# First loads of 128 partitions in the order of need, from two queues, and the first pair's splits in pieces with part of them on GpSimd

## The chip, the cores and the metric

The kernel runs on one core of a Trainium2 chip. The metric is the device time of one execution in microseconds (us), lower is better; a time stands for the median of several runs.

## What is computed

Attention over 4 batches of 8 heads with 576 positions and head size 64, then two feed-forward layers over the 2304 tokens:

```python
scores = scale * q @ k.T                      # 576 x 576 for each head
thresh = max(scores, axis=-1) - tau
scores = where(scores >= thresh, scores, -1e9)
attn = exp(scores - max(scores)); attn = attn / (sum(attn) + 1e-09)
x = attn @ v                                  # heads side by side: 2304 x 512
for w_in, w_out, act in layer 1, layer 2:     # 512 x 2048, 2048 x 512
    h = x @ w_in
    g = h - tanh(h)   (layer 1)   or   h * sigmoid(h)   (layer 2)
    x = g @ w_out
```

All data is float32. To keep precision at the rate of the `fp32r` form, every matmul operand is split into two parts: "hi", a copy that ScalarE rounds to `fp32r`, and "lo", the raw value minus hi.

## The kernel before, in words

**Attention.** The 32 heads are worked in 16 pairs (4 pairs a batch). A pair has 9 tiles of queries (`TILES`): tiles 0 to 7 hold 128 queries of one head each, heads in turn (tile 0 is head 0, tile 1 head 1, tile 2 head 0 again), tile 8 the last 64 queries of both heads. `steps(B, ks, first)` exists on TensorE, VectorE, ScalarE and GpSimd; it walks step numbers `k`, and what belongs to tile `q` happens at a fixed lag behind (`L_S` = 8 for the scores, `L_EXP` = 9, `L_SUM` = 10, `L_NORM` = 11, `L_T` = 13 for the transposes). These lags are the hand-written order of the work.

For each tile, TensorE computes the scores (L718: k_lo then k_hi, each over two halves of 288 keys, four matmuls; tile 8 has eight) into one of two PSUM buffers. VectorE reads them twice: a pass that scales and takes the row's maximum (L552), the statistics (L568) and the pass that applies the threshold (L584, which increments `lift_done` and so frees the scores' buffer). ScalarE takes the exponential (L421), VectorE the sum's reciprocal (L561, L577), GpSimd multiplies (L346), TensorE transposes the tile (L740), ScalarE copies that to SBUF (L407), and TensorE multiplies by v (L683).

**Where keys and queries come from.** They lie in HBM with the 64 features of a head first. Each raw tile `k_raw[u]`, `q_raw[u]` has 128 partitions: the same 64 rows twice, since the stationary operand `q_parts[u]` holds q_hi in partitions 0 to 63 and q_lo in 64 to 127, against k_hi or k_lo in both halves. The source holds the 64 rows once, so SyncE (SP in the profile) loads every raw tile by two DMAs of 64 partitions: `load_first` (L280) for the first pair, head by head, keys before queries, and `load_qk` (L273) for the later pairs, both heads in one. The load of tau (L264) goes ahead of them all. `load_qk` of pair 2 waits until the first pair is split (`qk_split`).

**The split of keys and queries.** In the steps of a pair its successor's keys and queries are split: hi on ScalarE (L432, L434), k_lo (L352) and q_lo (L361, partitions 64 to 127 alone) on GpSimd. The first pair has nobody before it: ahead of its steps ScalarE makes k_hi and q_hi of head 0, then of head 1 (L438, L439), each head after all four DMAs of that head, and VectorE makes k_lo and q_lo in the same order (L591, L595). Each of these eight instructions covers all 576 positions. Ahead of them VectorE computes a handful of constants from tau (L521 to L531). TensorE waits for the two lo parts of a head (`qk_split` at 2, then at 4) before tile 0 and tile 1:

```python
            for h in range(2):
                dve.wait_ge(k_hi_done, h + 1)
                dve.tensor_tensor(k_lo[0][:, h], ...).then_inc(qk_split, 1)
                dve.wait_ge(q_hi_done, h + 1)
                dve.tensor_tensor(rows, ...).then_inc(qk_split, 1)
```

**The layers.** Weights come in by 32 DMAs (L305) and are split on ScalarE, VectorE and GpSimd. Tokens go through in chunks of 512 (the last of 256); for each chunk and layer TensorE makes 16 hidden tiles (L761) and projects them (L777), three matmuls for each product of two split operands. ScalarE applies the activation (L471, L474), VectorE forms and splits g (L614, L619, L621). The output leaves at the end of each chunk of layer 2.

## Time and profile before

| | before |
|---|---|
| median of 3 runs | 1100.23 us (1100.09 to 1100.81) |
| the profiled execution's own time | 1100.23 us |
| its span (first to last instruction) | 1098.4 us |
| PE, PEld busy | 1076.1 us (98%), 870.5 us (79%) |
| DVE, ACT, POOL busy | 559.1 us (51%), 402.8 us (37%), 265.5 us (24%) |
| DMA | 46.38 MB, mean 42 GB/s |

PE is TensorE's matmuls, PEld its weight loads, DVE VectorE, ACT ScalarE, POOL GpSimd, SP SyncE. The profile's times are microseconds from the start of the span; 1.83 us of the execution lie outside the span. The 16 attention pairs take about the first 305 us, the two layers the rest.

### The profile page before, as it was taken

To read this page: it belongs to the slowest core of one execution; us is meant where nothing else is said; L and a number is where in the kernel's file an instruction comes from. 1 tells how busy PE (TensorE), PEld (TensorE's weight loads), DVE (VectorE), ACT (ScalarE), POOL (GpSimd) and SP (SyncE) were. 2 spreads that over 40 slices of the span, in tenths; PEclk is the share of its full clock that TensorE was granted. 3 is DMA by queue.
4 is the path that set the end of the run, shared out by engine and by line. 5 is a ranking of instruction groups with operands and counts; after the bars stand their busy time and mean duration, and the time that the engine had idled before them with its cause. 6 is when DMAs were issued, how large, how long until landed. Compare 5 with 4: busy or idle time off the path is not lost.

```text
span 1098.4 us, 15693 instructions
## 1 busy us (share of the span) xinstructions
PE 1076.1 (98%) x5808; PEld 870.5 (79%) x5808; DVE 559.1 (51%) x1342; ACT 402.8 (37%) x830; POOL 265.5 (24%) x240
## 2 busy tenths in 40 slices
PE   5999999999999999999999999999999999999998
PEld 4667677676678888888888889888888888888898
DVE  7999999999767543343343344622322322222222
ACT  5889898888732211121121121422211211111111
POOL 3767676776254200000000000444000000000000
PEclk9999999999999999999999999999999999999999
DMA  6334242431142100000000000232100000010010
GB/s 153 81 74 111 57 111 66 102 89 36 58 147 96 58 1 1 1 0 0 0 0 0 0 1 1 89 111 70 39 1 1 28 10 0 0 38 0 0 39 20
DMA packets 15195, 46.38 MB, mean 42 GB/s; under 512 B 2080, under 2 KB 2592, under 8 KB 15136
## 3 DMA queue, kind: packets, MB, share of 16 engines
q1 hardware_dynamic: 15136, 45.62, 14.8%
q8 instruction: 34, 0.56, 0.2%
q14 instruction: 25, 0.20, 0.1%
HBM read 40.89 MB, written 4.72 MB: 42 GB/s over the span
## 4 chain that ended last, share of the span: by engine, by line
PE 95%; DVE 1%; ACT 1%; POOL 0%; issue 0%; DVEq 0%; ACTq 0%
PE hid L761 36%; PE acc L777 35%; PE scores L718 9%; PE pv L683 8%; PE tps L740 6%; DVE x_lo L605 0%; ACT w_parts L450 0%; ACT x_hi L459 0%; DVE probs L584 0%; DVE probs L552 0%; ACT pT L407 0%; POOL q_parts L361 0%; DVE w_parts L635 0%; DVE stats L568 0%; ACT pR L409 0%
## 5 line engine op out<-in xcount | busy, mean ns | idle before, releaser
L761 PE MATMUL hid<-x_hi,w_parts 128*128 128x512 f32 (+1 forms) x1280 | 384.9, 368 | 3.2 <-DVE x_lo L605 2.1
L777 PE MATMUL acc<-g_hi,w_parts 128*128 128x512 f32 (+1 forms) x1280 | 384.1, 368 | 0.0
L761 PEld LDWEIGHTS hid<-x_hi,w_parts 128*128 128x128 f32 x1280 | 234.2, 189 | 44.6 <-DVE x_lo L605 2.2
L777 PEld LDWEIGHTS acc<-g_hi,w_parts 128*128 128x128 f32 x1280 | 234.1, 189 | 39.9
L761 PE MATMUL hid<-x_lo,w_parts 128*128 128x512 f32 (+1 forms) x640 | 235.4, 368 | 0.0
L777 PE MATMUL acc<-g_lo,w_parts 128*128 128x512 f32 (+1 forms) x640 | 235.4, 368 | 0.0
L619 DVE CAST g_hi<-h_act 128x512 fp32r<-128x512 f32 (+1 forms) x160 | 71.2, 445 | 270.0 <-ACT h_act L474 267.3
L374 POOL TENSOR_TENSOR w_parts<-w_raw,w_parts 128x1024 fp32r<-128x1024 f32 x30 | 73.6, 2457 | 400.0 <-ACT w_parts L450 399.9
L614 DVE TENSOR_TENSOR h_act<-hid,h_act 128x512 f32<-128x512 f32 (+1 forms) x80 | 51.0, 638 | 200.8 <-ACT h_act L471 200.8
L471 ACT ACTIVATE h_act<-hid 128x512 f32<-128x512 f32 (+1 forms) x80 | 44.4, 555 | 293.3 <-PE hid L761 293.3
L474 ACT ACTIVATE h_act<-hid 128x512 f32<-128x512 f32 (+1 forms) x80 | 44.4, 555 | 290.0 <-PE hid L761 290.0
L777 PEld LDWEIGHTS acc<-g_lo,w_parts 128*128 128x128 f32 x640 | 120.7, 189 | 19.9
L761 PEld LDWEIGHTS hid<-x_lo,w_parts 128*128 128x128 f32 x640 | 120.6, 189 | 19.9
L346 POOL TENSOR_SCALAR probs<-probs,rinv 128x576 f32<-128x576 f32 x144 | 107.4, 750 | 87.5 <-DVE rinv L577 78.4
L621 DVE TENSOR_TENSOR g_lo<-h_act,g_hi 128x512 fp32r<-128x512 f32 (+1 forms) x160 | 125.1, 782 | 5.5
L552 DVE TENSOR_SCALAR_CACHE_REDUCE probs<-scores,fine 128x576 f32<-128x576 f32 x144 | 116.8, 811 | 11.6 <-PE scores L718 11.3
L718 PE MATMUL scores<-k_lo,q_parts 128*128 128x288 f32 x336 | 106.8, 341 | 14.4 <-DVE q_parts L595 9.6
L718 PEld LDWEIGHTS scores<-k_lo,q_parts 128*128 128x128 f32 x336 | 64.0, 193 | 68.3 <-issue 39.7
L584 DVE SCALAR_TENSOR_TENSOR probs<-scores,stats,probs 128x576 f32<-128x576 f32 x144 | 117.8, 818 | 0.1
L421 ACT ACTIVATE probs<-probs,stats 128x576 f32<-128x576 f32 x144 | 111.2, 772 | 5.7 <-DVE probs L584 5.3
L407 ACT ACTIVATE pT<-tps 128x512 f32<-128x512 f32 x144 | 85.7, 595 | 31.5 <-PE tps L740 30.6
L740 PE MATMUL tps<-ident,probs 128*128 128x128 f32 x656 | 97.0, 276 | 0.0
(46 smaller groups left out, 765.9 us busy)
## 6 DMA issues: line engine op xcount, KB each, us to landing
w_raw<-w_in SPq DMA_DIRECT2D x32, 512.0 KB, 3.4
k_raw<-k_in SPq DMA_DIRECT2D x30, 288.0 KB, 4.8
q_raw<-q_in SPq DMA_DIRECT2D x30, 288.0 KB, 5.9
v_all<-v_in SPq DMA_DIRECT2D x16, 320.0 KB, 3.1
out<-xT SPq DMA_DIRECT2D x4, 1024.0 KB, 4.2
k_raw<-k_in SPq DMA_DIRECT2D x4, 144.0 KB, 3.0
q_raw<-q_in SPq DMA_DIRECT2D x4, 144.0 KB, 2.9
out<-xT SPq DMA_DIRECT2D x1, 512.0 KB, 2.9
```

Source lines behind the costliest of these rows:

```text
L346: pool.tensor_scalar(tile, tile, r, 1.0, ALU.mult, ALU.mult).then_inc(norm_done, 1)
L374: pool.tensor_tensor(w_parts[f][:, 1], w_raw[f % 2][:], w_parts[f][:, 0].bitcast(F32), ALU.subtract).then_inc(w_split, 1)
L407: last = act.activation(dst, src, ACT.Copy)
L421: act.activation(tile, tile, ACT.Exp, bias=stats[:, c, 0:1], scale=-SCALE / FINE, accum_out=rowsum[:, c:c + 1]).then_inc(exp_done, 1)
L552: dve.tensor_scalar(tile, scores[q % SBUFS][:, :, 0:HALF], fine[:], None, ALU.mult, ALU.max, accum_out=finemax[:, c:c + 1]).then_inc(max_d ...
L584: dve.scalar_tensor_tensor(out=tile, in0=scores[q % SBUFS][:, :, 0:HALF], scalar=stats[:, c, 1:2], in1=tile, op0=ALU.is_lt, op1=ALU.subtra ...
L621: dve.tensor_tensor(g_lo[s][:, 0:w], g, g_hi[s][:, 0:w].bitcast(F32), ALU.subtract).then_inc(g_split, 1)
L683: last = pe.matmul(pv[h * DH:(h + 1) * DH, 0:HALF], v_of(u, c, h), keys[c][h], start=(c == 0), stop=(c == FULL))
L718: last = pe.matmul(scores[q % SBUFS][:, a, c0:c0 + w], rows, keys, start=(i == 0), stop=(i == len(todo) - 1))
L740: last = pe.matmul(bank[:, c, :], block, ident[:], is_transpose=True, start=True, stop=True)
L761: last = pe.matmul(hid[f % HBANKS][:, 0:w], a, b[:, kc, 0:w], start=(kc == 0 and i == 0), stop=(kc == KC - 1 and i == 2))
L777: last = pe.matmul(acc[n][:, 0:w], a, b[f % GRING][:, 0:w], start=(f == 0 and i == 0), stop=(f == FT - 1 and i == 2))
```

## The change

What it does:

- The source arrays of keys and queries hold the 64 feature rows twice (`np.concatenate([rows, rows])` on the host), and every load of keys or queries is one DMA of 128 partitions instead of two of 64. This holds for all 16 pairs.
- The first pair's keys are loaded head by head by SyncE, and its queries in four pieces: the first 128 positions of head 0, the first 192 of head 1 (its layout has the last 64 queries in front), then the rest of head 0 (448) and of head 1 (384). The first piece and tau are loaded from ScalarE's own queue, the others from SyncE's, after both heads' keys.
- ScalarE splits k_hi of head 0, the first piece, k_hi of head 1, the second piece, then the other two, each behind its own DMA's semaphore.
- VectorE makes only k_lo of both heads and q_lo of the first piece. GpSimd makes q_lo of the other three pieces, ahead of its steps and after VectorE's three.
- TensorE waits before tiles 0 and 1 for VectorE's parts, and before tiles 1, 2 and 3 for GpSimd's pieces one, two and three.
- `qk_split` now counts the later pairs alone; its thresholds shift by 4. The load for pair 2 waits for the first pair's six lo instructions.

**SyncE and ScalarE, from the start of the program.** Of the loads before (rows of SP):

```order
L264 DMA tau<-tau_in 128x1
L280 DMA k_raw<-k_in 64x576 x2
L280 DMA q_raw<-q_in 64x576 x2
L280 DMA k_raw<-k_in 64x576 x2
L280 DMA q_raw<-q_in 64x576 x2
L273 DMA k_raw<-k_in 64x1152 x2
L273 DMA q_raw<-q_in 64x1152 x2
L287 DMA v_all<-v_in 128x640
```

and now (rows of SP):

```order
L288 DMA k_raw<-k_in 128x576 x2
L289 DMA q_raw<-q_in 128x192
L291 DMA q_raw<-q_in 128x448
L291 DMA q_raw<-q_in 128x384
L283 DMA k_raw<-k_in 128x1152
L283 DMA q_raw<-q_in 128x1152
L298 DMA v_all<-v_in 128x640
```

with these on ScalarE (rows of ACT, its table load behind two DMA issues):

```order
L407 DMA q_raw<-q_in 128x128
L408 DMA tau<-tau_in 128x1
L467 ACT_TABLE_LOAD
L467 ACTIVATE k_hi<-k_raw 128x576 [waits k_first0]
L463 ACTIVATE q_parts<-q_raw 128x128 [waits q_first0]
L467 ACTIVATE k_hi<-k_raw 128x576 [waits k_first1]
L463 ACTIVATE q_parts<-q_raw 128x192 [waits q_first1]
L463 ACTIVATE q_parts<-q_raw 128x448 [waits q_later0]
L463 ACTIVATE q_parts<-q_raw 128x384 [waits q_later1]
```

The first head's keys have nothing ahead of them on SP any more, and two DMAs stand where four stood in each head's place; tau and 128 positions of the queries have moved to ScalarE's queue.

**VectorE and GpSimd, up to the first tile.** VectorE before (rows of DVE):

```order
L531 TENSOR_TENSOR stat_bias<-margin,tau_low 128x1 [waits tau_steps]
L591 TENSOR_TENSOR k_lo<-k_raw,k_hi 128x576 [waits k_hi_done,tau_steps]
L595 TENSOR_TENSOR q_parts<-q_raw,q_parts 64x576 [waits q_hi_done]
L591 TENSOR_TENSOR k_lo<-k_raw,k_hi 128x576 [waits k_hi_done]
L595 TENSOR_TENSOR q_parts<-q_raw,q_parts 64x576 [waits q_hi_done]
L552 TENSOR_SCALAR probs,finemax<-scores,fine 128x576 [waits scores_done]
```

and now, VectorE first and then GpSimd:

```order
L562 TENSOR_TENSOR stat_bias<-margin,tau_low 128x1 [waits tau_steps]
L622 TENSOR_TENSOR k_lo<-k_raw,k_hi 128x576 [waits k_hi_done,tau_steps]
L627 TENSOR_TENSOR q_parts<-q_raw,q_parts 64x128 [waits first_q_hi]
L622 TENSOR_TENSOR k_lo<-k_raw,k_hi 128x576 [waits k_hi_done]
L583 TENSOR_SCALAR probs,finemax<-scores,fine 128x576 [waits scores_done]
```

```order
L340 AFFINE_SELECT ident<-ident 128x128
L383 TENSOR_TENSOR q_parts<-q_raw,q_parts 64x192 [waits consts_ready,first_q_hi,first_by_dve]
L383 TENSOR_TENSOR q_parts<-q_raw,q_parts 64x448 [waits first_q_hi]
L383 TENSOR_TENSOR q_parts<-q_raw,q_parts 64x384 [waits first_q_hi]
L357 TENSOR_SCALAR probs<-probs,rinv 128x576 [waits first_by_pool,rinv_done]
```

VectorE's second q_lo is gone from in front of its first pass over scores and its first is 128 positions wide instead of 576; GpSimd has three subtractions ahead of its first multiplication. TensorE's instructions are the same in the same order, with other waits.

The diff:

```diff
--- before.py
+++ after.py
@@ -36,6 +36,10 @@
 GROUP = 1
 
 
+FIRST = slice(0, P), slice(0, P + REST)
+LATER = slice(P, SEQ), slice(P + REST, SEQ)
+
+
 L_S = 8
 L_EXP = L_S + 1
 L_SUM = L_S + 2
@@ -222,7 +226,13 @@
         tau_steps = sem("tau_steps")
         ident_zero = sem("ident_zero")
         consts_ready = sem("consts_ready")
-        qk_first = sem("qk_first")
+        pads_zero = sem("pads_zero")
+        k_first = [sem(f"k_first{h}") for h in range(2)]
+        q_first = [sem(f"q_first{h}") for h in range(2)]
+        q_later = [sem(f"q_later{h}") for h in range(2)]
+        first_q_hi = sem("first_q_hi")
+        first_by_dve = sem("first_by_dve")
+        first_by_pool = sem("first_by_pool")
         qk_loaded = [sem(f"qk_loaded{u}") for u in range(2)]
         v_loaded = [sem(f"v_loaded{u}") for u in range(2)]
         k_hi_done = sem("k_hi_done")
@@ -261,23 +271,24 @@
 
         @block.sync
         def _(sp):
-            sp.dma_start(tau[:], tau_in).then_inc(tau_loaded, 16)
-
             def load_qk(B, p):
                 g = PAIRS * B + p
                 u = g % 2
-                if g >= 2:
-                    sp.wait_ge(qk_split, 4 * (g - 1))
+                if g == 2:
+                    sp.wait_ge(first_by_dve, 3)
+                    sp.wait_ge(first_by_pool, 3)
+                if g > 2:
+                    sp.wait_ge(qk_split, 4 * (g - 2))
                 for raw, src in ((k_raw[u], k_in), (q_raw[u], q_in)):
-                    for rows in (slice(0, DH), slice(DH, P)):
-                        sp.dma_start(raw[rows], src[:, bass.ds(g * 2, 2), :]).then_inc(qk_loaded[u], 16)
+                    sp.dma_start(raw[:], src[:, bass.ds(g * 2, 2), :]).then_inc(qk_loaded[u], 16)
 
             def load_first():
 
                 for h in range(2):
-                    for raw, src in ((k_raw[0], k_in), (q_raw[0], q_in)):
-                        for rows in (slice(0, DH), slice(DH, P)):
-                            sp.dma_start(raw[rows, h], src[:, h, :]).then_inc(qk_loaded[0] if h else qk_first, 16)
+                    sp.dma_start(k_raw[0][:, h], k_in[:, h]).then_inc(k_first[h], 16)
+                sp.dma_start(q_raw[0][:, 1, FIRST[1]], q_in[:, 1, FIRST[1]]).then_inc(q_first[1], 16)
+                for h in range(2):
+                    sp.dma_start(q_raw[0][:, h, LATER[h]], q_in[:, h, LATER[h]]).then_inc(q_later[h], 16)
 
             def load_v(B, p):
 
@@ -352,16 +363,27 @@
                         pool.tensor_tensor(k_lo[u][:, h], k_raw[u][:, h], k_hi[u][:, h].bitcast(F32),
                                            ALU.subtract).then_inc(qk_split, 1)
                     if what == "queries":
-                        pool.wait_ge(q_hi_done, 2 * g + h + 1)
+                        pool.wait_ge(q_hi_done, 2 * (g - 1) + h + 1)
 
                         if not first or k >= L_NORM:
                             pool.wait_ge(norm_done, STEPS * B + k - L_NORM + 1)
-                        pool.wait_ge(qk_split, 4 * g + 2 + h)
+                        pool.wait_ge(qk_split, 4 * (g - 1) + 2 + h)
                         rows = q_parts[u][DH:P, h, 0:SEQ]
                         pool.tensor_tensor(rows, q_raw[u][DH:P, h], rows.bitcast(F32),
                                            ALU.subtract).then_inc(qk_split, 1)
-                        pool.wait_ge(qk_split, 4 * g + 3 + h)
+                        pool.wait_ge(qk_split, 4 * (g - 1) + 3 + h)
                         pool.sem_inc(pool_waited, 1)
+
+            pool.wait_ge(consts_ready, 1)
+            pool.sem_inc(pool_waited, 1)
+            pool.wait_ge(first_by_dve, 3)
+            for i, (h, cols) in enumerate(((1, FIRST[1]), (0, LATER[0]), (1, LATER[1]))):
+                pool.wait_ge(first_q_hi, i + 2)
+                rows = q_parts[0][DH:P, h, cols]
+                pool.tensor_tensor(rows, q_raw[0][DH:P, h, cols], rows.bitcast(F32),
+                                   ALU.subtract).then_inc(first_by_pool, 1)
+            pool.wait_ge(first_by_pool, 3)
+            pool.sem_inc(pool_waited, 1)
 
             steps(0, range(STEPS), True)
             for B in range(1, BATCH):
@@ -382,6 +404,9 @@
 
         @block.scalar
         def _(act):
+            act.dma_start(q_raw[0][:, 0, FIRST[0]], q_in[:, 0, FIRST[0]]).then_inc(q_first[0], 16)
+            act.dma_start(tau[:], tau_in).then_inc(tau_loaded, 16)
+
             def steps(B, ks, first):
                 def here(q):
                     return q < STEPS and (q >= 0 or not first)
@@ -426,17 +451,23 @@
                     if what == "keys":
                         if h == 0:
 
-                            act.wait_ge(qk_loaded[u], 64 * (g // 2 + 1))
+                            act.wait_ge(qk_loaded[u], 32 * ((g + 1) // 2))
                             if not first or p >= 2:
                                 act.wait_ge(scores_done, TILES * (g - 1))
                         act.activation(k_hi[u][:, h], k_raw[u][:, h], ACT.Copy).then_inc(k_hi_done, 1)
                     if what == "queries":
                         act.activation(q_parts[u][:, h, 0:SEQ], q_raw[u][:, h], ACT.Copy).then_inc(q_hi_done, 1)
 
+            def first_queries(loaded, h, cols):
+                act.wait_ge(loaded, 16)
+                act.activation(q_parts[0][:, h, cols], q_raw[0][:, h, cols], ACT.Copy).then_inc(first_q_hi, 1)
+
             for h in range(2):
-                act.wait_ge(qk_loaded[0] if h else qk_first, 64)
+                act.wait_ge(k_first[h], 16)
                 act.activation(k_hi[0][:, h], k_raw[0][:, h], ACT.Copy).then_inc(k_hi_done, 1)
-                act.activation(q_parts[0][:, h, 0:SEQ], q_raw[0][:, h], ACT.Copy).then_inc(q_hi_done, 1)
+                first_queries(q_first[h], h, FIRST[h])
+            for h in range(2):
+                first_queries(q_later[h], h, LATER[h])
 
             steps(0, range(STEPS), True)
             for B in range(1, BATCH):
@@ -482,7 +513,7 @@
                                    ACT.Copy).then_inc(acc_by_act, 1)
 
             steps(BATCH - 1, range(STEPS, X_AT), False)
-            act.wait_ge(qk_split, 4 * PAIRS * BATCH)
+            act.wait_ge(qk_split, 4 * (PAIRS * BATCH - 1))
             split_x(0, 0, CHUNK)
             steps(BATCH - 1, range(X_AT, W_AT), False)
             weights_hi(0, 0)
@@ -515,7 +546,7 @@
 
             for u in range(2):
 
-                dve.memset(q_parts[u][:, 0, SEQ:640].bitcast(F32), 0.0).then_inc(consts_ready, 1)
+                dve.memset(q_parts[u][:, 0, SEQ:640].bitcast(F32), 0.0).then_inc(pads_zero, 1)
 
             dve.wait_ge(tau_loaded, 16)
             dve.tensor_scalar(tau_ok[:], tau[:], 0.0, None, ALU.is_ge).then_inc(tau_steps, 1)
@@ -589,10 +620,12 @@
             for h in range(2):
                 dve.wait_ge(k_hi_done, h + 1)
                 dve.tensor_tensor(k_lo[0][:, h], k_raw[0][:, h], k_hi[0][:, h].bitcast(F32),
-                                  ALU.subtract).then_inc(qk_split, 1)
-                dve.wait_ge(q_hi_done, h + 1)
-                rows = q_parts[0][DH:P, h, 0:SEQ]
-                dve.tensor_tensor(rows, q_raw[0][DH:P, h], rows.bitcast(F32), ALU.subtract).then_inc(qk_split, 1)
+                                  ALU.subtract).then_inc(first_by_dve, 1)
+                if h == 0:
+                    dve.wait_ge(first_q_hi, 1)
+                    rows = q_parts[0][DH:P, 0, FIRST[0]]
+                    dve.tensor_tensor(rows, q_raw[0][DH:P, 0, FIRST[0]], rows.bitcast(F32),
+                                      ALU.subtract).then_inc(first_by_dve, 1)
 
             steps(0, range(STEPS), True)
             for B in range(1, BATCH):
@@ -647,7 +680,8 @@
 
         @block.tensor
         def _(pe):
-            pe.wait_ge(consts_ready, 3)
+            pe.wait_ge(consts_ready, 1)
+            pe.wait_ge(pads_zero, 2)
 
             def steps(B, ks, first):
                 def here(q):
@@ -692,9 +726,11 @@
                         p, j = q // TILES, q % TILES
                         u, g, n = p % 2, PAIRS * B + p, STEPS * B + q
                         if first and q < 2:
-                            pe.wait_ge(qk_split, 2 * q + 2)
-                        elif j == 0:
-                            pe.wait_ge(qk_split, 4 * g + 4)
+                            pe.wait_ge(first_by_dve, 2 + q)
+                        if first and 0 < q < 4:
+                            pe.wait_ge(first_by_pool, q)
+                        if g > 0 and j == 0:
+                            pe.wait_ge(qk_split, 4 * g)
                         if not first or q >= SBUFS:
                             pe.wait_ge(lift_done, n - SBUFS + 1)
                         flat = q_parts[u][:].rearrange("p h s -> p (h s)")
@@ -810,8 +846,8 @@
     def features_first(x):
         x = by_pair(x)
         one = np.concatenate([x[:, :, 1, FULL * P:], x[:, :, 1, :FULL * P]], axis=2)
-        return np.ascontiguousarray(np.stack([x[:, :, 0], one], axis=2).transpose(4, 0, 1, 2, 3)
-                                    .reshape(DH, -1, SEQ))
+        rows = np.stack([x[:, :, 0], one], axis=2).transpose(4, 0, 1, 2, 3).reshape(DH, -1, SEQ)
+        return np.concatenate([rows, rows])
 
     q_in, k_in = features_first(q), features_first(k)
 
```

## Rows read from the trace of the kernel before

**Rows 1.** The page: busy tenths in 40 slices; the chain that ended last.
```profile
PE   5999999999999999999999999999999999999998
PEclk9999999999999999999999999999999999999999
PE 95%; DVE 1%; ACT 1%; POOL 0%; issue 0%; DVEq 0%; ACTq 0%
```

**Rows 2.** Chain of waits in order of time, to 36 us: start, length, what.
```profile
25.50 1.41 POOL q_parts L361
...
32.62 0.79 DVE probs L584
...
33.46 0.81 PE scores L718 x4
34.26 0.44 PE tps L740 x4
34.70 0.64 PE pv L683 x4
```

**Rows 3.** Timeline, 0 to 24 us: start, length, engine, line, what, [idle before <-releaser].
```profile
0.75 0.41 SPq L264 DMA_DIRECT2D tau<-tau_in  x1
1.22 1.19 SPq L280 DMA_DIRECT2D k_raw<-k_in  x2
...
2.83 0.15 DVE L521 TENSOR_SCALAR tau_ok<-tau 128x1 f32<-128x1 f32 x1 [1.81 <-DMA tau<-tau_in]
...
3.48 0.16 DVE L531 TENSOR_TENSOR stat_bias<-margin,tau_low 128x1 f32<-128x1 f32 x1
...
6.11 0.68 ACT L438 ACTIVATE k_hi<-k_raw 128x576 fp32r<-128x576 f32 x1 [4.08 <-DMA q_raw<-q_in]
...
6.90 0.76 DVE L591 TENSOR_TENSOR k_lo<-k_raw,k_hi 128x576 fp32r<-128x576 f32 x1 [3.26 <-ACT k_hi L438]
...
7.69 0.76 DVE L595 TENSOR_TENSOR q_parts<-q_raw,q_parts 64x576 fp32r<-64x576 f32 x1
...
8.59 0.58 PE L718 MATMUL scores<-k_lo,q_parts 128*128 128x288 f32 x1 [8.59 <-DVE q_parts L595]
...
9.45 0.44 PE L718 MATMUL scores<-k_hi,q_parts 128*128 128x288 f32 x1
10.09 0.76 DVE L595 TENSOR_TENSOR q_parts<-q_raw,q_parts 64x576 fp32r<-64x576 f32 x1
...
10.88 0.82 DVE L552 TENSOR_SCALAR_CACHE_REDUCE probs<-scores,fine 128x576 f32<-128x576 f32 x1
...
12.73 0.81 DVE L552 TENSOR_SCALAR_CACHE_REDUCE probs<-scores,fine 128x576 f32<-128x576 f32 x1
...
12.87 0.61 PE L718 MATMUL scores<-k_lo,q_parts 128*128 128x288 f32 x1 [0.64 <-DVE probs L584]
...
15.93 0.75 POOL L346 TENSOR_SCALAR probs<-probs,rinv 128x576 f32<-128x576 f32 x1 [14.45 <-DVE rinv L577]
...
24.16 0.29 PE L718 MATMUL scores<-k_hi,q_parts 128*128 128x288 f32 x1
```

**Rows 4.** Windows: stretch, length, PE, PEld, DVE, ACT, POOL busy, PEclk, DMA share, GB/s.
```profile
3.00:6.00 3.00, 0.00 (x0) 0.00 (x0) 0.58 (x9) 0.00 (x0) 0.00 (x0) 1.00 0.78 231
51.30:52.30 1.00, 1.00 (x11) 0.83 (x11) 1.00 (x6) 1.00 (x3) 1.00 (x1) 1.00 0.92 342
```

**Rows 5.** DMA issues: KB of one, median us from issue to landing (tau's: first 6 us).
```profile
v_all<-v_in SPq DMA_DIRECT2D x16, 320.0 KB, 3.1
tau<-tau_in SPq DMA_DIRECT2D x1, 0.5 KB, 2.1
```

**Rows 6.** Groups of instructions by form: busy us, mean ns of one | idle before.
```profile
L374 POOL TENSOR_TENSOR w_parts<-w_raw,w_parts 128x1024 fp32r<-128x1024 f32 x30 | 73.6, 2457 | 400.0 <-ACT w_parts L450 399.9
L361 POOL TENSOR_TENSOR q_parts<-q_raw,q_parts 64x576 fp32r<-64x576 f32 x30 | 42.5, 1417 | 10.6 <-ACT q_parts L434 10.0
L413 ACT ACTIVATE pR<-tps 64x64 f32<-64x64 f32 x32 | 7.0, 220 | 0.6
```

## The prediction

> **What bounds the kernel now.** I read the page first, then the chain that ended last, then the timeline of the start. The page shows TensorE busy nine tenths or more in every slice of the span but the first and the last, and 95% of the final chain on it [rows 1]. So it is the bound from some point on, and before that point something else is. The chain in order of time says where: from 33.46 us on TensorE follows on TensorE (scores, transposes, products with v); just before it stands VectorE's second pass over a tile, and at 25.50 us, where the traced chain begins, a GpSimd subtraction of 1.41 us [rows 2]. A change to the first 11 us can only move this point. It is worth what it moves the start of the tiles, as long as everything between hangs on that start.
>
> The timeline shows what that start hangs on [rows 3]. ScalarE waits until 6.11 us for the four DMAs of head 0. Then comes k_hi 0.68, k_lo on VectorE from 6.90 for 0.76, q_lo from 7.69 for 0.76, and TensorE's first matmul at 8.59; its tile ends at 9.45 + 0.44 = 9.89. VectorE takes that tile only at 10.88, for it first makes head 1's q_lo (10.09 to 10.85). From there the passes follow in rounds of 1.85 (10.88 to 12.73): TensorE's third tile starts at 12.87, on the pass that frees its buffer, and the first multiplication on GpSimd at 15.93, 5.05 behind VectorE's first pass. **The number that counts is 10.88, VectorE's first pass over scores.**
>
> **The landing of the first keys.** Call it T. Before, tau's issue held SP for 0.41 and the first keys were issued at 1.22; now they are issued at 0.75, where tau's issue stood [rows 3]. What has to land for tile 0 is k of head 0 (128 rows x 2304 B = 295 KB) and 128 queries (66 KB), together 360 KB where there were 590. How fast? In 3 to 6 us the loads of 64 partitions moved 231 GB/s with the DMA engines busy 0.78; while a v load of 128 partitions lands they move 342 GB/s [rows 4]. The nearest row in form is that v load: 328 KB in 128 partitions land 3.1 us after issue, against 2.1 for tau, which has next to no bytes [rows 5]. So 1.0 us for 328 KB, 0.9 for the keys, 0.2 for the queries that interleave with them: T = 0.75 + 2.1 + 0.9 + 0.2 = 3.95, I take **3.9**. Ends: without any share for the queries and with v's fixed part a little shorter 3.6; at 231 GB/s throughout, 0.75 + 2.1 + 1.56 = 4.4. The Trainium skill prices a transfer at 2 us plus its bytes at 436 GB/s (SBUF — State Buffer, the DMA setup-cost knee); by that T would be 0.75 + 2 + 0.83 = 3.6 and the gain below 0.3 larger. The same rule gives the v load 2.75 us where the trace has 3.1, so this trace is slower than the rule.
>
> **From T to the first pass.** k_hi 0.68, 0.11 to VectorE, k_lo 0.76, 0.03, then q_lo of 128 positions. VectorE's slope is (0.76 - 0.16) / 575 = 1.04 ns a position from L595 and the one-column L531 [rows 3], so 0.29. TensorE starts 0.14 later (8.45 to 8.59) and its tile takes 1.30 as before. Sum: 0.68 + 0.11 + 0.76 + 0.03 + 0.29 + 0.14 + 1.30 = 3.31, and a few hundredths to VectorE. First pass at 3.9 + 3.3 = **7.2 instead of 10.88: 3.7 us earlier.**
>
> **What must not be late beside it** (each with the time by which it may slip):
> - ScalarE before k_hi: two DMA issues now stand ahead of its table load. No row has an issue on ScalarE; SP's take 0.4 (tau) and 0.6 each (1.19 for two) [rows 3]. 0.75 + 0.6 + 0.4 + 1.3 of table load = 3.05, 0.9 ahead of T. Twice as long issues would still end at 4.0.
> - tau: issued at about 1.4, landed by 2.1 more at 3.5, and VectorE's constants take 2.83 to 3.64 = 0.81 more: 4.3, needed at T + 0.79 = 4.7. Slack 0.4, the smallest; see the first rival.
> - k of head 1 lands 0.9 behind T (1.3 at 231 GB/s). ScalarE takes it after head 0's queries (0.11 + 0.9 ns x 128 = 0.28 by L438 and the 64-column row [rows 3, 6], so from T + 0.97), done by T + 1.65 to 1.98; VectorE makes k_lo from T + 1.9 to 2.0, done by T + 2.75 at the latest. The pass comes at T + 3.3. Slack 0.55.
> - GpSimd's pieces: it waits for VectorE's three, so it starts at T + 2.85. Its price is (2457 - 1417) / 448 = 2.3 ns a position and 0.08 [rows 6]: 0.53, 1.12 and 0.97 for 192, 448 and 384. It ends at T + 3.4, 4.5 and 5.5. Tile 1 then starts about 0.1 later than tile 0 ends, at T + 3.5, and is done at T + 4.8; VectorE wants it one round after its first pass. A round is 1.85, so at T + 5.15. Tile 2 is freed then too, and tile 3 a round later, T + 7.0. Slack 0.35, 0.6 and 1.5. ScalarE's first exponential comes at T + 5.2, behind its last piece.
> - Pair 1's loads: they stood behind 8 half DMAs and stand behind 5 whole ones; bytes ahead are the same, the rate no lower. Pair 2's wait for six lo instructions that end at 9.4 instead of 10.85, 1.5 earlier for a pair that is wanted 3.7 earlier. Its keys are split ten steps after the first tile's, so some 18 us after the first pass, and its 1.18 MB take 5.1 at 231 GB/s: covered. Fewer issues on SP in later pairs: nothing, SP waits there for v's buffer to come free.
> - What lies after: GpSimd's subtraction at 25.50 and VectorE's rounds hang on the same start, so they move with it.
>
> The sum is against the profiled execution, which took 1100.23 us, 1098.4 of it span, and is itself the median: 1100.23 - 3.7 = **1096.5 us**. A change under 0.2% (2.2 us) could not be told from none here.
>
> **Rivals.**
> 1. *tau comes late.* It is issued behind the first queries on ScalarE's queue, and both queues feed the same DMA engines. If it gets its turn only among head 1's keys, it lands at T + 0.9 (1.2 at the low rate), the constants end at T + 1.7 (2.0), and k_lo of head 0 starts there and not at T + 0.79. All behind it, head 1's k_lo too, moves 0.9 to 1.2. The gain is 2.8, or 2.1 with T = 4.4 as well: 1097.4 to 1098.2. The Trainium skill says that each engine goes round its queues packet by packet (DMA: Bandwidth & Descriptors, queues, rings and completion order), which is this case. For it: no row before has a second queue. Against it: a row of tau is 4 bytes, and alone it took 2.1.
> 2. *The head start is lost on the way.* Something between 7 and 30 us does not move with the start (tile 1 late by its small slack, loads for pair 1, a stall at the hand-over to GpSimd) and takes 1 to 3.7 of it: 1097.5 to 1100.2.
> 3. *Slower: TensorE's clock rises later.* The page shows the granted clock full all along [rows 1], yet a scores matmul takes 0.44 us at 9 to 12 us and 0.29 at 24 us [rows 3], so the engine worked at the lower of its levels (1.2 GHz, not 2.4) at first and rose in between, when scores and transposes filled it. Now it starts earlier, but if it stayed low into the part where it is the bound, the work of a step there (0.81 + 0.44 + 0.64 at the upper level, [rows 2]) costs 1.9 more for each step. Two steps eat the gain of 3.7; it is slower by over 2.2 from a bit over three. Four give 1100.2 - 3.7 + 7.6 = 1104.1. Against it: the transposes that filled the engine come with the same lags behind the start, and the clock rose 10 us ahead of that part.
> 4. *It does not do what it says.* The order of instructions shows the moved loads and splits, so this can only be a second queue that costs start-up outside the span (1.83 us now) as much as it gives; no row prices that. It would be 1099 to 1101.
>
> **How the numbers follow.** My forecast (gain 3.3 to 4.1) has 0.62; tau late 0.18; head start partly lost 0.10; slower by the clock 0.04; start-up 0.06. Faster by over 0.2% is time below 1098.0: all of the forecast, most of tau's case (0.16) and half of the second rival's (0.05), so 0.83. Slower by over 0.2%: 0.04. Within: 0.13. The range goes from T = 3.6 with the runs' own spread (1095.9) to tau late with the low rate (1098.2).
>
> **What would show it.** k_hi of head 0 at 3.9 and not 6.11; the first matmul near 5.9, VectorE's first pass near 7.2, GpSimd's first multiplication near 12.2, and the chain's hand-over to TensorE near 29.8 instead of 33.46. If the first k_lo waits for the constants and not for k_hi, it is rival 1. If the first pass is early and the hand-over is not, rival 2. If matmuls of 0.44 stand after 23 us, rival 3. Wrong altogether would be a k_hi later than 5.

## The result, and the profile after

The changed kernel takes 1098.53 us (median of 18 runs) against 1100.32 before (18 runs): ratio 0.9983 [0.9976, 0.9990]. I had forecast 1096.5, range 1095.9 to 1098.2. It is faster, the interval lies wholly below 1, but the gain is 1.8 us (0.17%) where 3.7 was forecast. That is less than the 0.2% from which the prediction calls a change faster, a case to which it gave 0.13, and the time lies 0.3 above the range.

Times compared to tenths below are medians of the executions with TensorE's mean granted clock at 0.999 or 1.000, since those at 0.998, which every kernel here has, take 1.5 us longer. By these medians the changed kernel takes **1098.4** (10 of 18), and the kernel before 1100.1 in that series and 1100.2 to 1100.3 in the later ones. The profiled execution of the changed kernel took 1098.13 us, span 1096.3: 2.1 less than before's 1100.23. It is the fastest of the 18, so its difference is 0.3 larger than that of the medians.

The timeline of the start, the changed kernel (answers to [rows 3]):

```profile
0.74 0.41 ACTq L407 DMA_DIRECT2D q_raw<-q_in  x1
...
0.75 0.87 SPq L288 DMA_DIRECT2D k_raw<-k_in  x2
...
1.18 0.46 ACTq L408 DMA_DIRECT2D tau<-tau_in  x1
...
4.00 0.68 ACT L467 ACTIVATE k_hi<-k_raw 128x576 fp32r<-128x576 f32 x1 [1.04 <-DMA k_raw<-k_in]
...
5.02 0.15 DVE L552 TENSOR_SCALAR tau_ok<-tau 128x1 f32<-128x1 f32 x1 [4.00 <-DMA tau<-tau_in]
...
5.67 0.16 DVE L562 TENSOR_TENSOR stat_bias<-margin,tau_low 128x1 f32<-128x1 f32 x1
5.87 0.76 DVE L622 TENSOR_TENSOR k_lo<-k_raw,k_hi 128x576 fp32r<-128x576 f32 x1
...
7.09 0.58 PE L754 MATMUL scores<-k_lo,q_parts 128*128 128x288 f32 x1 [7.09 <-DVE q_parts L627]
...
8.43 0.82 DVE L583 TENSOR_SCALAR_CACHE_REDUCE probs<-scores,fine 128x576 f32<-128x576 f32 x1 [0.69 <-PE scores L754]
...
12.35 0.58 PE L754 MATMUL scores<-k_lo,q_parts 128*128 128x288 f32 x1 [0.54 <-DVE probs L615]
...
13.48 0.74 POOL L357 TENSOR_SCALAR probs<-probs,rinv 128x576 f32<-128x576 f32 x1 [3.02 <-DVE rinv L608]
```

k_hi begins at 4.00: the keys landed where I put them (3.9). But the first k_lo does not begin behind it at 4.79. It begins at 5.87, behind the constants, whose first instruction waited for tau until 5.02. VectorE's first pass over scores comes at 8.43 and not at 7.2.

Its chain in order of time, at the hand-over to TensorE (answers to [rows 2]):

```profile
23.02 1.41 POOL q_parts L372
24.48 0.81 PE scores L754 x4
...
30.98 0.81 PE scores L754 x4
31.79 0.44 PE tps L776 x4
```

The first pass is 2.45 us earlier than before (10.88 to 8.43), the GpSimd subtraction 2.48, the hand-over 2.48 (33.46 to 30.98). Nothing is lost on the way. The page still has 95% of the chain on TensorE. But the span is shorter by 2.1 only, so 0.4 went after that. The timeline of the last microseconds shows where, before and then changed:

```profile
1094.28 0.76 DVE L626 COPY xT<-acc 128x256 f32<-128x256 f32 x2 [3.15 <-PE acc L777]
1095.11 0.40 SPq L318 DMA_DIRECT2D out<-xT  x1
```

```profile
1091.79 0.76 DVE L659 COPY xT<-acc 128x256 f32<-128x256 f32 x2 [3.15 <-PE acc L813]
1093.01 0.40 SPq L329 DMA_DIRECT2D out<-xT  x1
```

The last copies start 2.49 earlier, the last store only 2.10: it is issued 0.83 behind their start before, 1.22 now.

So there were two things to test: that tau's lateness cost 1.2 us at the start, and that something on SyncE costs 0.4 at the end.

### The profile page after: what moved, and what is told of

Read it like the earlier page. It is cut to its first block, busy times and chain, and to the rows that moved or that the text cites. A ratio compares the mean times of both kernels' runs of the same rounds, so it can differ in the third digit from the quotient of the medians.

```text
span 1096.3 us, 15672 instructions
## 1 busy us (share of the span) xinstructions
PE 1076.1 (98%) x5808; PEld 870.7 (79%) x5808; DVE 557.6 (51%) x1341; ACT 403.0 (37%) x832; POOL 267.3 (24%) x243
## 4 chain that ended last, share of the span: by engine, by line
PE 95%; DVE 1%; ACT 1%; POOL 0%; issue 0%; DVEq 0%; ACTq 0%
PE hid L797 36%; PE acc L813 36%; PE scores L754 9%; PE pv L717 8%; PE tps L776 6%; DVE x_lo L638 0%; ACT w_parts L481 0%; ACT x_hi L490 0%; DVE probs L615 0%; DVE probs L583 0%; ACT pT L432 0%; POOL q_parts L372 0%; DVE w_parts L668 0%; DVE stats L599 0%; ACT pR L434 0%
```

## The experiments

Each ratio is against the kernel before, timed beside it on the same chip; "less than the changed kernel" compares with the 1098.4 above, from another series. That is good to about 0.2 us, the spread of the kernel before between the series. A start is read from one profile each: in the four runs whose first loads are issued just as in the changed kernel's (that kernel, e2, e5, e7) the first keys land at 3.97 to 4.04 and tau at 4.99 to 5.15, so 0.15 between two starts says nothing.

**Tau ahead of the queries on ScalarE's queue** (e1_tau_ahead)

```diff
-            act.dma_start(q_raw[0][:, 0, FIRST[0]], q_in[:, 0, FIRST[0]]).then_inc(q_first[0], 16)
             act.dma_start(tau[:], tau_in).then_inc(tau_loaded, 16)
+            act.dma_start(q_raw[0][:, 0, FIRST[0]], q_in[:, 0, FIRST[0]]).then_inc(q_first[0], 16)
```

> The changed kernel with ScalarE's two loads in the other order: tau, then the first 128 queries. In the changed kernel tau landed 3.8 us after its issue (at 4.98) and VectorE's constants, and with them k_lo of head 0, began behind it. Theory (tau had to take its turn behind the queries and among the keys): alone at the head of the queue it lands 2.1 us after issue, near 2.9; the constants are done by 3.8, k_lo of head 0 begins behind k_hi at 4.8, the first pass over scores comes at 7.3 instead of 8.43, and the time falls by 1.1 us from the changed kernel's. Rival (the second queue itself starts late, whatever is on it): tau lands at about 4.1, as the queries did, the constants are done at 4.95, the first pass comes at 7.45: 1.0 less. Rival (tau was not what counted): the first pass stays at 8.4 and the time too.

Measured: ratio 0.9981 [0.9972, 0.9990], 1097.95 where the changed kernel has 1098.4. My number for tau was wrong. Its timeline:

```profile
0.74 0.42 ACTq L407 DMA_DIRECT2D tau<-tau_in  x1
...
4.58 0.68 ACT L467 ACTIVATE k_hi<-k_raw 128x576 fp32r<-128x576 f32 x1 [1.62 <-DMA k_raw<-k_in]
4.77 0.15 DVE L552 TENSOR_SCALAR tau_ok<-tau 128x1 f32<-128x1 f32 x1 [3.75 <-DMA tau<-tau_in]
...
8.18 0.82 DVE L583 TENSOR_SCALAR_CACHE_REDUCE probs<-scores,fine 128x576 f32<-128x576 f32 x1 [0.69 <-PE scores L754]
```

First on its queue, issued at 0.74, tau still lands only just before 4.77, 0.2 behind the first keys. The DMA queues over 2.0 to 3.5 us show what it does meanwhile (q1 is SyncE's queue, q10 ScalarE's; packets, MB, share of the 16 engines). In this run:

```profile
q1 hardware_dynamic: 101, 0.22, 66.9%
q10 hardware_dynamic: 88, 0.00, 3.1%
```

and in the changed kernel, over the same stretch and then over 3.5 to 4.7 us:

```profile
q1 hardware_dynamic: 155, 0.33, 63.6%
q10 hardware_dynamic: 143, 0.06, 14.6%
```

```profile
q1 hardware_dynamic: 286, 0.37, 97.5%
q10 hardware_dynamic: 145, 0.00, 7.1%
```

88 packets with next to no bytes go beside 101 of the keys, nearly one for one; the changed kernel has 143 of the queries beside 155 and then 145 of almost nothing, tau's 4-byte rows, among the second keys. So in these two runs a row of 4 bytes waited its turn behind a row of 2304, and tau landed with the load whose rows it alternated with. The semaphores say the same. Each load raises its own in 16 steps, and it has landed with the last: in this run tau's steps come at 3.49 to 4.75 us, 0.19 behind those of head 0's keys (3.30 to 4.56), in the changed kernel at 4.49 to 4.99, 0.19 behind those of head 1's (4.31 to 4.80). The second queue is not late to start, which was the rival: its first packet starts at 2.02 us, 0.25 behind SyncE's.

By the Trainium skill each engine goes round its queues packet by packet (DMA: Bandwidth & Descriptors, queues, rings and completion order). The traces agree that turns are taken. The page puts 9 to 17 descriptors into a typical packet; here the turns are shorter than that: by 3.00 us 92 rows of keys and 62 of tau have started, some 6 and 4 to an engine, and neither load's semaphore has taken a step.

Two things do not fit a simple rule. The first keys land 0.58 later in this run (4.58 against 4.00) though tau has almost no bytes: from the lines above (16 engines x 1.5 us x share / packets) a row of keys took an engine 159 ns where it took 98 beside the queries. Why is open, and with one profile it may be this execution alone. So even an early tau would have given about 4.58 + 3.3 = 7.9 and not the 7.3 that I expected. And in e3 and e6 below, where the second queue started ahead of SyncE's (36 packets against 6 by 2.00 us in e3), tau lands at 4.96 and 4.94 while head 1's keys land at 5.53 and 5.37: which rows meet seems to depend on which queue starts first.

**The constants moved behind VectorE's three subtractions, tau as late as before** (e2_constants_late)

```diff
-            dve.wait_ge(tau_loaded, 16)
-            dve.tensor_scalar(tau_ok[:], tau[:], 0.0, None, ALU.is_ge).then_inc(tau_steps, 1)
...
+            dve.wait_ge(tau_loaded, 16)
+            dve.tensor_scalar(tau_ok[:], tau[:], 0.0, None, ALU.is_ge).then_inc(tau_steps, 1)
...
             steps(0, range(STEPS), True)
```

> The changed kernel with VectorE's constants from tau moved behind both k_lo and the first q_lo; loads unchanged. Theory: k_lo of head 0 begins at 4.8 behind k_hi, q_lo of 128 ends at 5.9, the first matmul comes at 6.0 (7.09 in the changed kernel), tile 0 is done at 7.3; k_lo of head 1 ends at 6.7 and the constants at 7.5, so the first pass comes at 7.5 instead of 8.43: 0.9 us less than the changed kernel, tau landing as late as before. If tau's wait was not what held k_lo, the first matmul stays at 7.1 and the time too.

Measured: ratio 0.9970 [0.9958, 0.9982], 1097.29: 1.1 us less than the changed kernel. Timeline:

```profile
4.01 0.68 ACT L467 ACTIVATE k_hi<-k_raw 128x576 fp32r<-128x576 f32 x1 [1.05 <-DMA k_raw<-k_in]
...
4.72 0.76 DVE L613 TENSOR_TENSOR k_lo<-k_raw,k_hi 128x576 fp32r<-128x576 f32 x1 [3.56 <-ACT k_hi L467]
...
5.95 0.58 PE L755 MATMUL scores<-k_lo,q_parts 128*128 128x288 f32 x1 [5.95 <-DVE q_parts L618]
...
6.51 0.15 DVE L622 TENSOR_SCALAR tau_ok<-tau 128x1 f32<-128x1 f32 x1
...
7.40 0.82 DVE L574 TENSOR_SCALAR_CACHE_REDUCE probs<-scores,fine 128x576 f32<-128x576 f32 x1
```

The keys land at the same time, k_lo follows k_hi, the first matmul comes at 5.95 and the pass at 7.40. With tau as late as before (its last step comes at 5.01), that shows the wait for tau to be what the start lost.

**Tau back at the head of SyncE's queue** (e8_tau_on_sp)

```diff
         @block.sync
         def _(sp):
+            sp.dma_start(tau[:], tau_in).then_inc(tau_loaded, 16)
...
-            act.dma_start(tau[:], tau_in).then_inc(tau_loaded, 16)
```

> The changed kernel with tau back at the head of SyncE's queue, the first 128 queries alone on ScalarE's. Theory (tau is late only by its turn in the second queue): it lands at 2.8 as before, the constants are done by 3.6; the first keys are issued 0.45 later, at 1.20, and land at about 4.4; k_lo begins behind k_hi at 5.2, the first pass comes at 4.4 + 3.3 = 7.7 instead of 8.43: 0.7 us less than the changed kernel (SyncE has one instruction more, which may or may not touch the last store). Rival (a second queue in use delays whatever is loaded): tau lands at 4 or later all the same.

Measured: ratio 0.9969 [0.9956, 0.9981], 1096.95, 1.4 less than the changed kernel. Timeline:

```profile
3.06 0.15 DVE L553 TENSOR_SCALAR tau_ok<-tau 128x1 f32<-128x1 f32 x1 [2.04 <-DMA tau<-tau_in]
...
4.19 0.68 ACT L468 ACTIVATE k_hi<-k_raw 128x576 fp32r<-128x576 f32 x1 [1.72 <-DMA k_raw<-k_in]
...
7.55 0.82 DVE L584 TENSOR_SCALAR_CACHE_REDUCE probs<-scores,fine 128x576 f32<-128x576 f32 x1 [0.60 <-PE scores L755]
```

Tau has landed by 3.06 and the keys, issued 0.45 later, land only 0.2 later. That gives 0.9 at the start, and the pass comes 3.36 behind k_hi's start, where the prediction's terms add to 3.3. Another 0.35 is the end of the program: the store comes 0.87 behind the copies' start, with one more instruction on SyncE. Together 1.2, the difference of the two profiled executions (1098.13 and 1096.95).

**Tau on SyncE's queue behind the first keys** (e9_tau_second)

```diff
-                for h in range(2):
-                    sp.dma_start(k_raw[0][:, h], k_in[:, h]).then_inc(k_first[h], 16)
+                sp.dma_start(k_raw[0][:, 0], k_in[:, 0]).then_inc(k_first[0], 16)
+                sp.dma_start(tau[:], tau_in).then_inc(tau_loaded, 16)
+                sp.dma_start(k_raw[0][:, 1], k_in[:, 1]).then_inc(k_first[1], 16)
...
-            act.dma_start(tau[:], tau_in).then_inc(tau_loaded, 16)
```

> The changed kernel with tau on SyncE's queue behind the first keys and ahead of the second ones; only the 128 queries stay on ScalarE's. Theory (a load lands with those whose turns it shares or follows): the first keys keep their place at 0.75 and land at 3.9, tau right behind them at about 4.1, the constants are done at 4.9, the first k_lo begins there (0.1 to 0.2 behind k_hi), and the first pass comes at 7.4; time 1096.8, about that of the run with tau at the head. Rival (4-byte rows cost a turn each and push the second keys back): k_hi of head 1 begins 0.3 or more later than in that run (5.47) and the pass stays at 7.6 or later.

Measured: ratio 0.9970 [0.9958, 0.9983], 1097.1. The instruction that waits for tau began at 4.41 (it landed 3.2 after issue, at 4.39, not 4.1), so k_lo began at 5.26 and the pass came at 7.83: 0.4 later than I had said. The rival had the late pass right but not the reason, for k_hi of head 1 began at 5.46 and not 0.3 later. Even behind one load of keys tau is too late for constants that stand ahead of k_lo.

**Later loads in halves again** (e3_later_halves)

```diff
-                    sp.dma_start(raw[:], src[:, bass.ds(g * 2, 2), :]).then_inc(qk_loaded[u], 16)
+                    for rows in (slice(0, DH), slice(DH, P)):
+                        sp.dma_start(raw[rows], src[rows, bass.ds(g * 2, 2), :]).then_inc(qk_loaded[u], 16)
```

> The changed kernel with the loads of pairs 1 to 15 back in two DMAs of 64 partitions each (the first pair's as changed). Theory: the later loads are covered, so the hand-over to TensorE stays at 31.0 us; SP has its instructions back, and if the last store's late issue (0.46 us behind VectorE's last copies instead of 0.07, with an instruction fetch there in the trace) came from where SP's instructions lie, it may come back to 0.07 and the time fall by 0.4. Rival: the 128-partition loads of pair 1 help the start; then the start gets later with them gone, by up to 1 us.

Measured: ratio 0.9978 [0.9969, 0.9987], 1097.89: 0.5 less. First pass 8.39 and hand-over 30.95, as in the changed kernel; the last store 0.83 behind the copies' start. The rival may be half true. Head 1's keys land at 5.53 where they land at 4.80 in the changed kernel; that costs nothing here, behind the wait for tau:

```profile
5.56 0.68 ACT L468 ACTIVATE k_hi<-k_raw 128x576 fp32r<-128x576 f32 x1 [0.48 <-DMA k_raw<-k_in]
```

**Sixteen idle waits on SyncE** (e7_sp_padded)

```diff
+            for _ in range(16):
+                sp.wait_ge(tau_loaded, 16)
             load_w(0, 0)
```

> The changed kernel with 16 waits of SyncE on tau's semaphore, long since reached, put in front of the weights' loads, and nothing else. Theory (the last store is issued 0.39 us later than before because an instruction block is fetched just then, and which instruction that hits depends on how many SyncE has before it): with about as many instructions as before back, the store is issued 0.83 us behind the start of the last copies and not 1.22, and the time falls by 0.4 to 0.5 (1097.9). Rival (it is the size or form of the loads, not the count): it stays at 1.22 and the time at 1098.4. The start is not touched either way.

Measured: ratio 0.9976 [0.9967, 0.9985], 1097.90, 0.5 less for instructions that do nothing, though its first pass was 0.15 later in the profile (8.58). Its last microseconds:

```profile
1093.38 0.76 DVE L661 COPY xT<-acc 128x256 f32<-128x256 f32 x2 [3.15 <-PE acc L815]
1094.21 0.40 SPq L331 DMA_DIRECT2D out<-xT  x1
```

So it is not the size or form of the loads; adding instructions to SyncE is enough. In all 13 traces the store comes either 1.22 behind the copies' start (the changed kernel, e1, e2, e5) or 0.83 to 0.87 (the other nine). In those four and in none of the other nine an instruction block of 8 KB is fetched 0.6 us after the start of the store's issue (e4 has one 2.6 us after it); the queue of these fetches over the changed kernel's last 5 us:

```profile
q14 instruction: 1, 0.01, 0.5%
```

The fetch comes after the delay, so it marks the place in the instruction stream and is not shown to be its cause. Which step of SyncE's loop exit takes the 0.39 stays open.

**Only the 128-partition loads** (e4_only_128)

```diff
-                        for rows in (slice(0, DH), slice(DH, P)):
-                            sp.dma_start(raw[rows, h], src[:, h, :]).then_inc(qk_loaded[0] if h else qk_first, 16)
+                        sp.dma_start(raw[:, h], src[:, h, :]).then_inc(qk_loaded[0] if h else qk_first, 16)
```

> The kernel before with one change: every load of keys or queries in one DMA of 128 partitions. Tau first, one queue, whole heads, all lo parts on VectorE. Theory: head 0 needs 590 KB, issued from 1.22 on, at some 350 GB/s instead of 231: landed at 1.22 + 2.1 + 1.7 = 5.0 instead of 6.1, head 1 some 1.7 behind, at 6.7 instead of 8.6. VectorE's first pass hangs on head 1's q_lo: 0.68 + 0.67 on ScalarE (or k_lo, q_lo at 0.76 each behind head 0's, from 5.9: 5.9 + 4 x 0.79 = 9.1), so 9.1 instead of 10.9: 1.8 us less than before. Rival (issue or HBM sets the rate, not the number of partitions): the first k_hi stays near 6.0 and the time within 0.3 us of before.

Measured: ratio 0.9991 [0.9982, 1.0000], 1100.02 against 1100.23: 0.2 us and not 1.8. Timeline:

```profile
4.92 0.68 ACT L436 ACTIVATE k_hi<-k_raw 128x576 fp32r<-128x576 f32 x1 [2.90 <-DMA q_raw<-q_in]
...
8.35 0.68 ACT L436 ACTIVATE k_hi<-k_raw 128x576 fp32r<-128x576 f32 x1 [2.17 <-DMA q_raw<-q_in]
...
10.64 0.82 DVE L550 TENSOR_SCALAR_CACHE_REDUCE probs<-scores,fine 128x576 f32<-128x576 f32 x1
```

Head 0 lands at 4.9 as forecast (6.1 before), but head 1, all of it issued by 3.04, at 8.32 and not at 6.7. The trace shows what held it. Its two loads raise their semaphore in 32 steps: 26 have come by 6.69, where I had put the landing, 31 by 7.76, and the last comes at 8.32. The rows of the first pair are 1.18 MB; the last of them ends at 7.96, and up to 8 us SyncE's queue had moved

```profile
q1 hardware_dynamic: 846, 1.73, 69.3%
```

so 0.5 MB of later loads went ahead of it. The engines do not get through their rows evenly, and a load lands with the last step. How late that is may well change from one execution to the next (there is one trace): the ten times behind this kernel's median run from 1099.56 to 1100.39, a spread of 0.8 where the changed kernel's is 0.4, and the profiled one, at 1100.26, is among the slowest. So the wide loads alone are worth 0.2 by the median, and up to 0.7 in one execution. What the change adds to them besides GpSimd's part (the order of need, the smaller first piece, the second queue) brings the first tile forward, by difference; no run has the new order with loads of 64 partitions, so the order's own share is not measured.

**GpSimd's pieces back on VectorE** (e5_no_pool)

```diff
-            pool.wait_ge(first_by_dve, 3)
-            for i, (h, cols) in enumerate(((1, FIRST[1]), (0, LATER[0]), (1, LATER[1]))):
-                pool.wait_ge(first_q_hi, i + 2)
...
+            for i, (h, cols) in enumerate(((1, FIRST[1]), (0, LATER[0]), (1, LATER[1]))):
+                dve.wait_ge(first_q_hi, i + 2)
...
```

> The changed kernel with GpSimd's three q_lo pieces given back to VectorE, behind its k_lo of head 1 and ahead of its first pass. Theory (the pieces are worth what they take VectorE in front of the first pass): 0.36 + 0.63 + 0.56 for 192, 448 and 384 positions at 1.04 ns each, and the last one waits for its data; in the changed kernel k_lo of head 1 ends at 7.73 and the pass comes at 8.43, so it comes at 7.73 + 1.6 = 9.3 and the time rises by 0.9 us. Rival (the pieces on GpSimd hold TensorE's tiles 1 to 3 back and their own gain is lost): the time stays within 0.3 of the changed kernel's.

Measured: ratio 0.9989 [0.9980, 0.9998], 1099.22, 0.85 more than the changed kernel. First pass 9.32 against 8.43. The three pieces take VectorE from 7.93 to 9.30; in the profile 0.15 of the later pass is tau's, which landed that much later. The part on GpSimd is worth 0.7 to 0.9 us, as its time on VectorE says.

**Late constants and halves together** (e6_late_and_halves)

> Both edits that helped, in one: constants behind the first k_lo, q_lo and k_lo (-1.0 us in the run of that edit) and the loads of pairs 1 to 15 in halves (-0.5). They act at opposite ends of the program, so they should add: first pass at 7.4 to 7.5, last store issued 0.83 us behind the start of the last copies, and 1.5 us less than the changed kernel (1096.9 where that has 1098.4). If the second edit's gain came from the start and not from the last store, they need not add, and it is 1.0 only.

Measured: ratio 0.9969 [0.9957, 0.9981], 1096.78: 1.6 less than the changed kernel, pass 7.59, store 0.83 behind. By the medians the two gains (1.1 and 0.5) add. The pass is 0.2 later than in e2, as head 1's keys land at 5.37, late as in e3, and the wait for tau no longer covers it.

**Late constants, tau as SyncE's fourth load** (e10_tau_fourth_late), on the kernel of e2:

```diff
-            act.dma_start(tau[:], tau_in).then_inc(tau_loaded, 16)
...
                 sp.dma_start(q_raw[0][:, 1, FIRST[1]], q_in[:, 1, FIRST[1]]).then_inc(q_first[1], 16)
+                sp.dma_start(tau[:], tau_in).then_inc(tau_loaded, 16)
```

> Constants behind VectorE's three subtractions, and tau as the fourth load of SyncE's queue; the 128 queries alone on ScalarE's. Theory: nothing small stands ahead of either head's keys now, so T is 3.9 at most, k_lo begins at 4.7, the second k_lo ends at 6.7, the constants at 7.5; first pass at 7.5. SyncE has one instruction more than in the changed kernel, as in the run with tau at its head, so the last store comes without the fetch: time 1096.9, equal to that run and 0.4 below the run with late constants alone. If the last store is late all the same, 1097.3.

Measured: ratio 0.9963 [0.9949, 0.9978], 1096.77. Its timeline has the k_hi and k_lo that I had forecast for the change, and the pass 0.3 later than 7.2, behind the constants:

```profile
4.08 0.68 ACT L467 ACTIVATE k_hi<-k_raw 128x576 fp32r<-128x576 f32 x1 [1.62 <-DMA k_raw<-k_in]
...
4.80 0.76 DVE L613 TENSOR_TENSOR k_lo<-k_raw,k_hi 128x576 fp32r<-128x576 f32 x1 [3.64 <-ACT k_hi L467]
...
7.48 0.82 DVE L574 TENSOR_SCALAR_CACHE_REDUCE probs<-scores,fine 128x576 f32<-128x576 f32 x1
```

It is 3.5 us under the kernel before of its own series (1100.31), where the changed kernel's gain is 1.8. It is the fastest here, though level with e6 and with the next one.

**One queue for all loads** (e11_one_queue): e10 with the first 128 queries as SyncE's second load, which makes tau the fifth.

> The same with the 128 queries on SyncE's queue too, behind the first keys: one queue for all loads, constants late. Theory (the second queue only saves an issue of 0.45 us on SyncE, and its load shares the keys' turns): the first keys land up to 0.2 earlier (3.7 to 3.9), the 128 queries 0.3 behind them, still ahead of k_lo's end, the second keys up to 0.4 later by the issue, and the first pass stays within 0.2 of 7.5; time within 0.3 of the two-queue version (1096.9). Rival (two queues are worth something here): first pass 0.5 or more later.

Measured: ratio 0.9965 [0.9952, 0.9977], 1096.87, 0.1 from e10. The first keys land at 3.70, 0.4 earlier with nothing alternating; the second keys' k_hi begins at 5.39 instead of 4.89, and the pass comes at 7.59. What the second queue saves in issue, it takes in turns: the two runs are level.

## Why the prediction was wrong

- **What bounds, and what the first 11 us are worth**: right. The shift of the first pass (2.45) arrives whole at the hand-over (2.48) and at the last copies (2.49). The second rival (lost on the way) did not happen. Nor did the third: the last scores matmul of 0.44 us starts at 20.51 us where it started at 22.72 before, so TensorE rose to its upper level 2.2 us earlier as well, ahead of the hand-over.
- **T**: right, 3.9 forecast, 4.00 measured, and no luck: it is 3.97 to 4.04 in the four profiles with these first loads. With 128 partitions the engines move 331 GB/s over 3 to 6 us, where they moved 231 [rows 4].
- **From T to the first pass**: 3.3 right as a sum of work: e2 has its first matmul 1.94 behind k_hi's start where the terms add to 2.01, and e8 its first pass 3.36 behind.
- **tau, "landed by 2.1 more at 3.5 ... Slack 0.4, the smallest": this is the step that failed.** I took the landing price of a load that had the engines to itself [rows 5] for one whose rows alternate with rows of keys. It landed 3.8 after issue, at 4.98. k_lo began 1.08 later than the forecast's 4.79, and the pass 1.2 later than 7.2. It was my first rival, in mechanism and size (landing at T + 0.9 said, T + 1.0 found; gain 2.8 said, 2.45 found at the start), and I gave it 0.18. The doubt I set against it, that a row of tau is 4 bytes, is the very thing that does not help: turns go by rows, not by bytes.
- **The end of the program**: no term at all. I looked at SyncE's issues in the later pairs, set them at nothing and stopped there. Fewer instructions on SyncE moved the last store by 0.39 to the wrong side (e7 gets it back). Without it 1098.53 would be 1098.1, just inside a range that reached to tau's case. The sum of both: 3.7 - 1.2 - 0.4 = 2.1, the profiled difference.
- **GpSimd's pieces, pair 1's and pair 2's loads, the issues on ScalarE**: right. The issues on ScalarE took 0.41 and 0.46, VectorE's rounds stay 1.85 (passes at 8.43, 10.28, 12.12), so no piece came too late for it, and the pieces took GpSimd 2.65 where I had 2.62. Pair 1's loads may have helped the start, which I had not said: in both runs with halves (e3, e6) head 1's keys land 0.4 to 0.7 us later than in the four profiles named above.

## What to carry to other kernels

Ask of each load on a second queue which rows it will alternate with, and put what a constant needs either ahead of the bulk on the same queue (e8) or its use behind the first work that does not need it (e2): the latter gave 1.1 us for moving nine lines. Width alone brought 0.2; a first load split by order of need, a smaller first piece and part of the work on an idle engine brought the rest. A load is there with the last of its 16 steps, so leave slack behind one on which the start hangs. When a gain of a microsecond or two is at stake, look at the last store too, and compare by where it stands behind the last copy.

## What I had not expected of the hardware

- A load of 512 bytes in 128 rows took 2.1 us to land at the head of the only queue, 3.2 behind the first keys on SyncE's (e9), 3.8 as second on ScalarE's queue and 4.0 as first on it, beside loads of keys on SyncE's.
- The last store's issue has two values, 0.83 to 0.87 and 1.22 us behind the start of the last copies; sixteen idle waits on SyncE moved it from the later to the earlier and were worth 0.5 us.
- A load of 128 partitions takes SyncE 0.43 us to issue where two of 64 took 1.19 to 1.24.
- With only the wide loads (e4), head 1's two loads landed 5.7 us after the issue of the second, at 8.32, though 31 of their 32 semaphore steps had come by 7.76 and half of them by 6.1.
